# An attention block with two feed-forward layers: raw keys and queries transposed for both heads at once, parts placed by DMA, reciprocals spread through DRAM, and an instruction order written out per tile

## What is computed

```
q, k, v: (4 batches, 8 heads, 1152 rows, 64)
q_pool = q.reshape(B, H, 576, 2, 64).mean(axis=3)
scores = q_pool @ k.T / 8;  scores -= scores.max(-1)
attn = exp(scores);  attn /= attn.sum(-1) + 1e-9
x = (attn @ v), heads side by side             # 2304 tokens x 512
h = x @ w_in                                   # 512 x 2048
g = where(h >= 1, h, where(h <= -1, 0, (h + 1)**2 / 4))
y = g @ w_out                                  # 2048 x 512
out = max(y @ w1, y @ w2, y @ w3) @ w2_out     # 512 x 768, 768 x 512
```

## Time and profile before

| | |
|---|---|
| median of 3 runs | 1293.17 us (1292.42 to 1294.87) |
| the profiled execution | 1294.91 us, span 1293.0 us |
| granted TensorE clock, mean | 0.996 of full speed |
| attention phase | from the start to 583.2 us |
| feed-forward phase | 583.2 us to the end, 1293.0 us |
| busy share over the span | PE 97%, DVE 59%, ACT 51%, POOL 26% |

### The profile page before, as it was taken

How to read it: one execution, slowest core, us unless ns; L and a number is a source line. 1 busy time by engine, 2 the same in 40 slices (tenths; PEclk the granted TensorE clock), 3 DMA queues, 4 the chain that set the end, 5 groups by cost and what they waited for, 6 DMA issues and landing times.

```text
span 1293.0 us, 21136 instructions
## 1 busy us (share of the span) xinstructions
PE 1259.6 (97%) x7876; PEld 1207.9 (93%) x7876; DVE 758.1 (59%) x1579; ACT 658.8 (51%) x1570; POOL 335.5 (26%) x332
## 2 busy tenths in 40 slices
PE   7999999999999999989999999999999999999998
PEld 6989899999989898979999999999999999999997
DVE  5888888888888888874544444444453222223221
ACT  5989899999989898962222222222222111111111
POOL 5343443444433444258600000000282000000000
PEclk9999999999999999989999999999999999999999
DMA  3111111111111111113300000000030000000000
GB/s 119 47 56 56 52 33 57 53 41 56 56 47 56 56 56 38 52 49 100 113 1 1 1 1 1 1 1 1 17 122 26 1 25 25 1 25 5 20 25 25
DMA packets 59140, 49.07 MB, mean 38 GB/s; under 512 B 2977, under 2 KB 48033, under 8 KB 59041
## 3 DMA queue, kind: packets, MB, share of 16 engines
q1 hardware_dynamic: 59040, 47.72, 12.1%
HBM read 42.99 MB, written 4.72 MB: 37 GB/s over the span
## 4 chain that ended last, share of the span: by engine, by line
PE 79%; ACT 18%; DVE 1%; issue 1%; POOL 1%; DMA 0%; SPq 0%; POOLq 0%; ACTq 0%
PE hid L868 33%; PE acc L900 16%; ACT probs L558 8%; PE trans L413 8%; ACT pT_hi L548 6%; PE acc L932 6%; PE scores L456 6%; PE values L475 5%; PE scores L458 4%; ACT kT L568 1%; ACT value_aux L582 1%; PE trans L424 1%; DVE qT L662 1%; ACT X L578 1%; ACT qT L571 1%
## 5 line engine op out<-in xcount | busy, mean ns | idle before, releaser
L626 DVE TENSOR_REDUCE neg_max_parts<-scores 128x1 f32<-128x384 f32 x432 | 234.7, 552 | 44.0 <-PE scores L458 30.3
L548 ACT ACTIVATE pT_hi<-trans 128x384 fp32r<-128x384 f32 x432 | 191.2, 491 | 55.8 <-PE trans L413 52.3
L640 DVE TENSOR_TENSOR pT_lo<-trans,pT_hi 128x384 fp32r<-128x384 f32 x432 | 212.0, 546 | 7.3 <-ACT pT_hi L548 6.3
L558 ACT ACTIVATE probs<-scores,neg_max 128x768 f32<-128x768 f32 (+1 forms) x288 | 212.0, 753 | 4.0 <-DVE neg_max L633 4.0
L456 PE MATMUL scores<-kT,qT 128*128 128x384 f32 x480 | 199.6, 416 | 9.4 <-ACT probs L558 9.1
L413 PE MATMUL trans<-ident,probs 128*128 128x128 f32 x1296 | 189.7, 273 | 9.6 <-DVE qT L662 6.4
L413 PEld LDWEIGHTS trans<-ident,probs 128*128 128x128 f32 x1296 | 157.5, 140 | 24.9 <-DVE qT L662 11.5
L868 PE MATMUL hid<-qT,w_slots 128*128 128x384 f32 x936 | 171.6, 336 | 0.0
L868 PE MATMUL hid<-x_hi,w_slots 128*128 128x384 f32 x624 | 167.6, 335 | 0.0
L868 PEld LDWEIGHTS hid<-qT,w_slots 128*128 128x128 f32 x936 | 163.7, 188 | 1.0
L986 ACT ACTIVATE excess<-rise,halves 128x384 f32<-128x384 f32 x96 | 59.2, 617 | 203.0 <-DVE rise L1070 203.0
(11 more groups left out here) (101 smaller groups left out, 1998.2 us busy)
## 6 DMA issues: line engine op xcount, KB each, us to landing
k_raw<-in_k SPq DMA_DIRECT2D x16, 576.0 KB, 4.0
v_raw<-in_v SPq DMA_DIRECT2D x32, 288.0 KB, 2.8
q_raw<-in_q SPq DMA_DIRECT2D x32, 256.0 KB, 3.0
out<-X SPq DMA_DIRECT2D x18, 256.0 KB, 2.8
q_raw<-in_moe_w_out SPq DMA_DIRECT2D x14, 256.0 KB, 3.1
k_raw<-in_moe_w SPq DMA_DIRECT2D x12, 256.0 KB, 3.1
k_raw<-in_moe_w_in SPq DMA_DIRECT2D x8, 256.0 KB, 2.9
k_raw<-in_moe_w_out SPq DMA_DIRECT2D x8, 256.0 KB, 3.0
```

Source lines behind the costliest of these rows:

```text
L548: act.activation(*tile_places(pT[0], src, t, g), ACT.Copy).then_inc(p_hi_done, 1)
L558: act.activation(probs[:, par, :].rearrange("p (n k) -> p n k", n=GROUPS)[:, ns[0]:ns[-1] + 1], scores[:, bank:bank + len(ns), 0:SB], ACT. ...
L626: dve.tensor_reduce(neg_max_parts[:, par, n:n + 1], scores[:, score_banks(u9)[n], 0:SB], AX_X, ALU.max, negate=True).then_inc(parts_done, 1)
L640: dve.tensor_tensor(*tile_places(pT[1], src, t, g), hi.bitcast(F32), ALU.subtract).then_inc(p_lo_done, 1)
```

## The change

**Order.** The three lists and `PREP` become tables with a line per tile, in which each group, bank and run of products is named with its tile (`T1.0`: group 0 of tile 1; `S3.0`: bank 0 of tile 3's scores; `W`: products of the pair before; `H`, `L`: high and low part; `K`, `Q`: next pair's keys and queries). The programs are written out for all 16 pairs.

```diff
-PE_ORDER = ["S1", "T0", "S2", "T1", "T2", "N0", "V", "X"]
-ACT_ORDER = ["T0", "T1", "T2", "E0", "E1", "X", "V"]
-DVE_ORDER = ["T0", "T1", "T2", "M0", "X", "M1", "M2"]
+PE_ORDER = """
...
+T4.0 S5.1 S5.2 T4.1 S6.0 T4.2 V0:0-4 V0:4-8 K1 K2 S6.1
...
+T7.0 S8.2 T7.1 S9.0 V1:8-13 V1:13-18 S9.1 T7.2 S9.2
...
```

```diff
+                src = k_heads[bass.ds(head(pair) + h, 1)].rearrange("h p (t d) -> p (h t) d", d=D)
+                sp.dma_start(k_raw[:, :, h, :], src).then_inc(k_loaded, 16)
...
+                src = k_raw[:, g * GK + j].rearrange("p h d -> p (h d)")
+                last = pe.transpose(trans[:, BANK[group], j * P:(j + 1) * P], src, ident[:])
...
+            act.activation(k_parts[:, 0, g * GK * P:(g + 1) * GK * P], trans[:, BANK["K", pair, g], 0:GK * P],
+                           ACT.Copy).then_inc(k_hi_done, 1)
...
+            dve.tensor_tensor(k_parts[:, 1, cols], trans[:, BANK["K", pair, g], 0:GK * P],
+                              k_parts[:, 0, cols].bitcast(F32), ALU.subtract).then_inc(k_lo_done, 1)
...
+        def place_k(pair):
+            sp.wait_ge(k_lo_done, pair * KG)
+            for h in range(2):
+                for a in range(2):
+                    copy_parts(sp, kT[rows_of(a), pair % 2, h, :], k_parts[rows_of(h), a, :], k_placed)
...
-                pe.wait_ge(k_evac, pair * KG + k_groups)
+            if n == 0 and t == 0 and pair > 0:
+                pe.wait_ge(k_placed, 64 * pair)
+                pe.wait_ge(q_placed, 128 * pair)
...
-                terms = [(0, 0), (1, 1)]
+                pe.matmul(out, hi, k_parts[:, 0, keys], start=True, stop=False)
+                pe.matmul(out, lo, k_parts[:, 0, keys], start=False, stop=False)
+                last = pe.matmul(out, hi, k_parts[:, 1, keys], start=False, stop=True)
```

```diff
-            act.activation(X[own, bass.ds(pair * SQ + half * HALF, HALF)], values[own, 0:HALF],
-                           ACT.Copy).then_inc(value_kept, 1)
-            act.activation(value_aux[own, :], values[other, 0:HALF], ACT.Copy).then_inc(value_kept, 1)
+            act.activation(value_all[:, n % 2, :], values[:, 0:HALF], ACT.Copy).then_inc(value_kept, 1)
...
+        for i in range(PAIRS):
+            if i > 0:
+                send_recips(i - 1)
+            if i + 1 < PAIRS:
+                place_q(i + 1)
+            if i + 2 < PAIRS:
+                sp.wait_ge(q_trans_done, (i + 1) * QG)
+                load_q(i + 2)
+            load_v(i, 1)
+            if i > 0:
+                move_values(i - 1, 2)
+                spread_recips(i - 1)
+                move_values(i - 1, 3)
+            if i + 1 < PAIRS:
+                load_v(i + 1, 0)
+            if i + 2 < PAIRS:
+                sp.wait_ge(k_trans_done, (i + 1) * KG)
+                load_k(i + 2)
+            if i + 1 < PAIRS:
+                place_k(i + 1)
+            else:
+                load_weights(0)
+                load_weights(1)
+            move_values(i, 0)
+            move_values(i, 1)
```

```diff
+            add_values(i, 0)
+            if i == PAIRS - 1:
+                split_weights(0)
+            add_values(i, 1)
+        add_values(PAIRS - 1, 2, split_weights(1))
+        add_values(PAIRS - 1, 3, split_weights(2))
+        for n in range(3, 8):
+            split_weights(n)
+        scale(PAIRS - 1)
```

More of the change, by code:

```diff
@@ L194, in attention_phase @@
[L194 to L209 removed]
+            return q_lo_done, (group[1] - 1) * QG + group[2] + 1
@@ L467, in value_products @@
+            last.then_inc(scores_done, 1)
+        def value_products(pair, n, products):
+            h, half = n // 2, n % 2
+            t = (2, M_TILE, 7, TILES - 1)[n]
             for m in products:
@@ L528, in pe_program @@
-        two_pairs(0, first=True)
-        for d in range(1, PAIRS // 2 - 1):
-            two_pairs(d)
-        two_pairs(PAIRS // 2 - 1, last=True)
-        for half in range(2):
-            start = VALUE_STEPS[TILES - 1][2].stop if half == 0 else 0
-            value_products(PAIRS - 1, 1, half, range(start, 2 * KT))
-        meanwhile(0)
-        for g in range(RG):
-            bank, before = RING_END[g]
-            wait_bank(before, PAIRS - 2)
-            prep_transposes(PAIRS, 0, "R", g, bank)
@@ L645, in scale_x, with tail, queries @@
+        def tail(par, bank, done):
+            for h in range(2):
+                last = scaled_rest(q_tail(qT_lo, par, h), trans[rows_of(h), bank, h * TAIL:(h + 1) * TAIL],
+                                   q_tail(qT_hi, par, h))
+            last.then_inc(done, 1)
+        def queries(pair, g):
+            dve.wait_ge(q_hi_done, (pair - 1) * QG + g + 1)
+            bank = BANK["Q", pair, g]
             if g == 0:
-                dve.wait_ge(add_done, pair * 4)
-                x = X[:, bass.ds(x0, 4 * P)]
@@ new lines, in dve_program @@
+        for kind, g in FIRST:
+            first_rest(kind, g)
+        for n in range(GROUPS):
+            tile_max(0, n)
+        for kind, g in SECOND:
+            first_rest(kind, g)
+        for n in range(GROUPS):
+            tile_max(1, n)
+        for pair in range(PAIRS):
+            for step in steps_of(DVE_ORDER):
+                kind = step[0]
+                if kind == "L":
+                    lo_of_tile(pair * TILES + step[1], step[2])
+                elif kind == "M" and pair * TILES + step[1] < ALL_TILES:
+                    tile_max(pair * TILES + step[1], step[2])
+                elif kind == "K" and pair + 1 < PAIRS:
+                    keys(pair + 1, step[1])
+                elif kind == "Q" and pair + 1 < PAIRS:
+                    queries(pair + 1, step[1])
+                elif kind == "R" and pair > 0:
+                    reciprocals(pair - 1)
@@ L942, in two_tiles1 @@
                 for f in range(C1):
-                    if not (first and u == 0 and f < EARLY):
-                        hidden1(pe, tile, f, u)
+                    hidden1(pe, tile, f, u)
                     if f >= LAG1:
```

957 lines of the change are left out of this document (477 added, 480 removed).

## The result

The changed kernel takes **1511.05 us** (1509.63 to 1516.73, 4 runs) against 1293.16 (1292.42 to 1294.87) in the runs beside it: ratio 1.169, 95% interval [1.166, 1.172]. 1257 had been predicted. The profiled execution has a span of 1515.0 us.

What follows compares the result with a forecast made beforehand. DVE was taken to bound each attention pair: 31.1 us plus 1.5 surplus and 0.2 key wait gave a 32.8 us pitch. From 1294.9, minus 33.0, plus 1.6 start, minus 5.6 passage made 1257.9, forecast 1257 us, range 1237 to 1285.

Steps and rivals of the forecast that it cites:

- Engine work: Attention, per pair after the change: PE 29.9 us, ACT 28.2, DVE 31.1, with DVE now the fullest engine.
- the pitch: Attention, time from pair to pair: 31.1 + 1.5 + 0.2 = 32.8 us, 2.13 less than before.
- the surplus: Attention, per pair: cost of hand-overs between engines above DVE's 31.1 us, taken as 1.5 us between 0.3 and 2.5.
- the passage: From last exponentials to first product with x: 5.5 us instead of 12.1; together with slot 2's loss, 5.6 us less.
- the placing of the keys: Next pair's keys, copied by SP's DMAs before its first score: PE waits 0.2 us per pair, ends 0 and 4.5.
- nothing in a pair's middle stands behind it: POOL in attention: its waits are now for DMAs, and no work in a pair's middle is held up by them.
- The copies: SBUF key copies, 1.18 MB per pair: 3.7 us on all 16 engines, 7.4 if 64 partitions engage half the path.
- rival 1: Key copies between 64 partitions run at half rate, PE stands 3.5 to 4.5 us per pair; 1317 us, chance 0.1.
- The issue price: SP's queue in attention: 30 DMAs per pair at 0.52 us each, 16 us of a pair's 33.
- Packets of 256 bytes: Key loads, 2304 packets: each costs between 13.3 ns and 26.6 ns, 1.9 to 3.8 us over 16 engines.
- the start: First key load with 256-byte packets, queries behind it: 1.6 us more (0 to 4), first cast at 6.8 us.
- Slot 2: Feed-forward weights at the passage: POOL splits slot 2 only after adding the moved values, so PE loses 1.5 us.

Runs made afterwards that it cites:

- queue_by_need: Changed kernel with only order altered: SP's DMAs placed where data are ready or the taker near, POOL averaging queries later; 1419.87 us.
- turned: queue_by_need with reciprocals' read-back behind the key placing, and reciprocals transposed on PE and copied by ACT so nine 512-byte rows go out; 1328.12 us.
- recips_in_rows: Changed kernel with reciprocals written as 128 rows of 36 bytes instead of 1152 4-byte elements, order of reciprocals wrong; 1439.49 us.
- four_bytes_back: early_queries with the reciprocals again written directly as 1152 packets of 4 bytes, without transpose and ACT copy; 1320.28 us.
- early_queries: turned with keys placed group by group in twelve copies, queries loaded and averaged earlier and placed by four DMAs instead of eight; 1276.75 us.
- turned_128: turned with keys placed by two copies over 128 partitions instead of four over 64, scores wrong; 1286.69 us.

## Why the prediction was wrong

**Engine work: right.** ACT 28.2 predicted, 28.06 measured; DVE 31.1, 30.55. With the DMAs out of the way the pitch is 33.24 against 32.8, and the surplus over DVE's 31.1 is 2.1 where 1.5 was taken. Even so the whole takes 1273.7 us and not 1257: 15.5 x 0.44 = 6.8 us of that are the pitch, 3.1 the passage (8.6 us from the last exponential, 552.34, to the first product with x, where 5.5 was predicted); the rest was not taken apart.

**The step that failed is the placing of the keys: its path over SP and POOL.** The prediction took 0.2 us of wait per pair; PE waited 10.0. It summed SP's issues (16 us of 33) and took nothing for SP's waits: "then SP issues four DMAs", 2.3 us after the transposes, with only the load directly ahead in view. But an in-order queue is late by each wait in it and by what is then still to be issued: parts ready at 384.30, first copy at 396.51. SP first stood 11.3 us per pair for the reciprocals, then issued for 13.5 us. Of the instructions behind that, two wait for POOL (v's split, the addition), and POOL waits for a DMA of SP's own. That "nothing in a pair's middle stands behind it" was said of POOL's waits for the moved values; v's split did, then SP, then the keys. Order alone (queue_by_need) gave 91 of the 218 us back.

**The write of the reciprocals was priced at nothing.** The instruction was in the diff, 1152 elements of 4 bytes, and no row of before resembled it; it should have had a bound. Written in packets of 36 bytes instead it gives back 72 us in the changed kernel, and turned on PE first, with everything else mended, 43.5 us.

**The copies: the wrong end.** 3.7 us was taken from a load over 128 partitions; 207 GB/s make 5.7 us, between that and the 7.4 of rival 1 (for the 0.5 us of landing there was no row either). In turned, where the order and the write are mended, PE still waits 2.2 us per pair for them. Rival 1 (1317 us, chance 0.1) had the side and a part of the cause, at a wait of 4 us; it lacked the queue and the write, and so does every case I had weighed.

**The issue price.** 0.52 us held only where little was queued. In the changed kernel an issue took up to 2.87 us in the pair shown, behind the 4-byte write; in recips_in_rows the same ones took 0.52 to 0.6. Twelve key copies took 13.22 us in four_bytes_back.

**Packets of 256 bytes.** 13.3 to 26.6 ns were bracketed, and the start was priced at 1.6 us. In early_queries, 321 to 324 us, with mostly the key load under way:

```profile
q1 hardware_dynamic: 2315, 0.70, 110.2%
```

1.102 x 3 x 16 / 2315 = 22.8 ns each, 2247 of them under 512 bytes (a share over 100% counts packets that overlap; by 100% it is 20.7 ns; the 68 larger packets are counted in both, so both are a little high). The rule of three fixed cycles (Trainium skill, DMA: Bandwidth & Descriptors, "Why small descriptors are slow") would have given 0.58 x 26.6 = 15.4; the measurement lies between that and one price per packet, 26.6. The first cast came at 6.05 us, 0.8 after the earlier trace rows, where 6.8 was predicted.

**The passage.** 10.8 us instead of 5.5: the prediction's sum goes over the last transposes, parts and value products and has no term for DVE's split of the tokens, which took 6.2 us and ended some 4 us after them. Slot 2 took 7.8 instead of 1.5: POOL waits 10.90 us for the moved values before it splits it, the queue once more; the prediction named this path and took it too short. In the feed-forward phase (794.47 us to the end, 720.5 us, limit given: 712) that wait is 7.8 of the 10.7 us more than before.

**The clock** was in no case. Where PE stood for 10 us it came back at half speed, 1.7 us in the pair shown; 15 times that, 26 us, is an estimate for all.

## What to carry to other kernels

Price an in-order DMA queue by walking it: for each instruction, when its data are there and what the one ahead of it waits for, and follow each wait through the other engines until it ends outside the queue; if it comes back, it is a loop and sets the pitch. Turn small elements into rows on a compute engine before they go out: one transpose and one copy of nine rows here are worth 43.5 us. Copies between 64 partitions are fine when issued piece by piece as the pieces are ready, and are not when a product waits for the last.

## What the runs showed of the hardware

- 1152 packets of 4 bytes from SBUF to DRAM took 11.06 us from issue to landing (queue_by_need) with 11.5% of the DMA engines' time used from 376 to 384 us. In four_bytes_back one issue behind them took 3.94 us, and twelve copies 13.22 us to issue instead of 8.69.
- SBUF copies between 64 partitions moved 207 GB/s (turned), over 128 partitions 365 GB/s (turned_128), with all 16 engines shown busy in both (103.6% and 102.6%): the busy share doesn't tell the rate.
- Packets of mostly 256 bytes from DRAM took 20.7 to 22.8 ns each (early_queries, 321 to 324 us).
- Most DMA issues by SP took 0.5 to 0.6 us; behind the 4-byte write single ones took 2.87 us (changed kernel) and 3.94 us (four_bytes_back).
- After 10.01 us without a product the granted clock was 0.50, and ten value products took 2.40 instead of 1.32 us; after 4.07 us it was 0.62.
- DVE's two instructions that split 128x1536 tokens took 0.95 and 1.76 us in the nine cases with POOL idle, and up to 2.82 and 3.83 us in the three beside POOL's splits of weights (changed kernel).
